# The first layer of an attention plus two-network kernel: seven block products of summed operands in place of eight

## The reference: what is computed

```python
# attention: q, k, v are (2, 8, 768, 64), proj is (64, 6)
mask = q_bucket[:, :, :, None] == k_bucket[:, :, None, :]     # buckets from signs of q @ proj, k @ proj
scores = where(mask, scale * q @ k.T, -1e9)
attn = exp(scores - max) / (sum + 1e-9)
x = (attn @ v) as 1536 tokens of 512
# first network: w1, w2 (512, 1024), w3 (1024, 1024), w_out (1024, 512)
x = ((x @ w1) * (x @ w2)) @ w3 @ w_out
# second network: w_gate, w_val (512, 1536), w_out (1536, 512)
out = (sigmoid(x @ w_gate) * (x @ w_val)) @ w_out
```

## Time and profile before

| | us |
|---|---|
| median of 3 runs (lowest, highest) | 790.92 (788.36, 793.75) |
| the profiled execution | 791.71 |
| its span, first to last instruction | 789.9 |
| busy in the span: PE, weight loads, DVE, ACT, POOL | 761.5, 699.9, 445.5, 426.1, 293.2 |
| matmuls | 4232 |
| mean granted clock of TensorE | 0.991 of full |

### The profile page before, as it was taken

One profiled execution on the slowest core, in us unless ns is written; L12 is line 12 of the kernel. 1 busy time (PEld: TensorE's weight loads), 2 busy tenths in 40 slices (PEclk: granted clock), 3 DMA queues, 4 the chain that ended last, 5 costly groups with the idle time before them and its releaser, 6 DMA issues.

```text
span 789.9 us, 12696 instructions
## 1 busy us (share of the span) xinstructions
PE 761.5 (96%) x4232; PEld 699.9 (89%) x4232; DVE 445.5 (56%) x995; ACT 426.1 (54%) x793; POOL 293.2 (37%) x203
## 2 busy tenths in 40 slices
PE   7889999999999988999999999999999999999998
PEld 4677878888797887999999999999999999988886
DVE  5879999999999997522222202534424415673100
ACT  5767888888888897423323323363453354624100
POOL 3777273645537243211112350024464464050000
PEclk9899999999999999999999999999999999999999
DMA  6592634435372600010000010001011010401101
GB/s 163 181 192 64 154 102 112 127 87 145 73 182 54 149 29 27 28 54 27 27 0 0 27 54 0 1 1 54 27 28 51 27 46 8 159 1 54 40 27 40
DMA packets 24653, 51.76 MB, mean 66 GB/s; under 512 B 3592, under 2 KB 9352, under 8 KB 24624
## 3 DMA queue, kind: packets, MB, share of 16 engines
q1 hardware_dynamic: 24400, 51.32, 24.1%
q10 hardware_dynamic: 224, 0.07, 0.0%
HBM read 29.43 MB, written 3.15 MB: 41 GB/s over the span
## 4 chain that ended last, share of the span: by engine, by line
PE 74%; DVE 10%; issue 5%; ACT 4%; DMA 3%; SPq 1%; POOL 1%; DVEq 0%; ACTq 0%; POOLq 0%
PE pair_bank L1183 12%; PE pair_bank L1184 12%; PE pair_bank L1185 12%; PE bank L1184 7%; PE bank L1183 7%; PE bank L1185 7%; PE bank L1108 5%; PE bank L1093 4%; PE pair_bank L1081 3%; DVE pt_lo L861 3%; DVE rowmax L828 3%; ACT pt_hi L550 2%; DVE prob L853 1%; DMA qk_raw<-in_qk 1%; DMA sq<-q_codes 1%
## 5 line engine op out<-in xcount | busy, mean ns | idle before, releaser
L861 DVE TENSOR_TENSOR pt_lo<-bank,pt_hi 128x384 fp32r<-128x384 f32 x192 | 97.6, 549 | 13.9 <-ACT pt_hi L550 13.6
L550 ACT ACTIVATE pt_hi<-bank 128x384 fp32r<-128x384 f32 x192 | 84.7, 488 | 34.7 <-PE bank L1093 33.4
L1093 PEld LDWEIGHTS bank<-ident,prob 128*128 128x128 f32 x576 | 67.4, 142 | 34.7 <-DVE pt_lo L861 14.5
L1093 PE MATMUL bank<-ident,prob 128*128 128x128 f32 x576 | 83.6, 280 | 14.8 <-DVE pt_lo L861 14.0
L568 ACT ACTIVATE prob<-pair_bank,ebias,escale 128x768 f32<-128x768 f32 x96 | 95.3, 992 | 4.2 <-DVE ebias L839 4.2
L1081 PE MATMUL pair_bank<-mk,sq 128*128 128x384 f32 x384 | 89.2, 354 | 5.5 <-DMA sq<-q_codes 3.0
L828 DVE TENSOR_REDUCE rowmax<-pair_bank 128x1 f32<-128x768 f32 x96 | 90.9, 947 | 4.3 <-PE pair_bank L1081 4.2
L1183 PE MATMUL pair_bank<-operand_hi,g_hi 128*128 128x384 f32 x240 | 80.3, 334 | 0.8 <-ACT u L550 0.8
L1185 PE MATMUL pair_bank<-operand_hi,g_lo 128*128 128x384 f32 x240 | 80.2, 334 | 0.0
L1081 PEld LDWEIGHTS pair_bank<-mk,sq 128*128 128x128 f32 x384 | 64.7, 190 | 15.2 <-issue 12.9
L444 POOL TENSOR_TENSOR w_lo<-w_raw,w_hi 128x512 fp32r<-128x512 f32 (+1 forms) x24 | 40.6, 1693 | 98.2 <-ACT w_hi L550 96.9
(11 more groups left out here) (163 smaller groups left out, 1963.7 us busy)
## 6 DMA issues: line engine op xcount, KB each, us to landing
sq<-hl SPq DMA_DIRECT2D x45, 192.0 KB
w_raw<-in_w SPq DMA_DIRECT2D x32, 256.0 KB, 2.8
mk<-hl SPq DMA_DIRECT2D x15, 384.0 KB
qk_raw<-in_qk SPq DMA_DIRECT2D x7, 768.0 KB, 5.3
v_raw<-in_v SPq DMA_DIRECT2D x16, 192.0 KB, 2.7
wo_raw<-in_wo SPq DMA_DIRECT2D x12, 256.0 KB, 3.9
out<-out_sb SPq DMA_DIRECT2D x12, 256.0 KB, 2.0
mk<-hl SPq DMA_DIRECT2D x15, 192.0 KB
```

Source lines behind the costliest of these rows:

```text
L550: return act.activation(dst, src, ACT.Copy)
L861: dve.tensor_tensor(pt_lo[(k // UQ) % 2][cut], t_bank[j][:, 0:384].rearrange("p (t n) -> p t n", t=3), pt_hi[(k // UQ) % 2][cut].bitcast(F ...
L1093: mm = pe.transpose(t_bank[j][:, 128 * t:128 * t + 128], prob[k % 3][:, 128 * (3 * j + t):128 * (3 * j + t) + 128], ident[:, :])
```

## The change

Layer 1 goes by the same seven products. Its eight groups are four pairs (`PAIRS1`), for `w1` and `w2`: eight units more, numbered 0 to 7, before layer 3's twelve. The helpers of layer 3 (`product`, `unit`, `kept`, `pair_weights`, `load_pair`) serve both. ACT's gate function is a plain copy in layer 1.

- The attention output `x_f` is now cut in blocks: B11 is pairs 4 and 5, B12 pairs 0 and 1 (T3 is made in its place), B22 pairs 2 and 3, B21 pairs 6 and 7. POOL makes T3 (two instructions of 128x768, one for each side) in the last but one pair, T2 and T1 in the last, DVE makes T4 after it.
- POOL also makes the first unit's weight sums (in the last but one pair) and their low part, its raw weights' low part and the high and low parts of B11 and the high part of T3 in the last pair. ACT makes that unit's high parts in steps 8 and 9 of the last but one pair, and three high parts of T2 and T1 in steps 9, 10 and 11 of the last. Gone are POOL's 128x1536 `x_hi` and `x_lo`, its split of the first 128x1024 weights, and ACT's 128x1024 `w_hi` at step 8 of the last pair.
- `h` stands whole in float32 (`h_f`). It is split only after its last piece, in six pieces: for the first chunk 128x2304 and 128x768, for the others 128x3072, high part by ACT (`h_high`), low part by DVE (`h_low`).
- In the last unit of layer 1 (7) ACT makes two high parts of `wp` between its `u1` and `u2` copies.
- The tiles of gate times value are three of 4 slices in place of one of 8 and one of 4, so their splits are 36 instructions of 128x512 on each engine, where 12 of 128x1024 and 12 of 128x512 were. ACT's and DVE's layer 3 loops are written out.

The core of the diff:

```diff
+X_HI_ORDER = ((T2, 0), (T2, 1), (T1, 0), (T1, 1), (B22, 0), (B21, 0), (B22, 1), (T4, 0), (B21, 1), (T4, 1))
+X_LOW_ORDER = ((T3, 0), (T3, 1), (T2, 0), (T1, 0), (T2, 1), (T1, 1), (B22, 0), (B22, 1), (B21, 0), (B21, 1),
+               (T4, 0), (T4, 1))
+PAIRS1, PAIRS3 = KF // 2, KF2 // 2
...
@@ POOL, pair(p, ...)
+                    else:
...
+                        x_sum(T2, T3, B11, ALU.add)
+                        pool.wait_ge(x_sums_done, 4)
+                        x_sum(T1, B22, T2, ALU.subtract)
                     attention_sum(p, 1)
                     v_split(p, 1)
+                if ahead:
+                    pool.wait_ge(x_done, PAIRS)
+                    for side in range(2):
+                        pool.tensor_tensor(x_raw(T3, side), x_raw(B22, side), x_raw(T3, side),
+                                           ALU.subtract).then_inc(x_sums_done, 1)
+                    pair_sums(0, 0)
...
-                    rounded(x_hi[:, 0, :, :], x_f[:, 0:KX, 0:HALF]).then_inc(x0_hi_done, 1)
-                    w_split(0, U1, w_raw[0][:, :])
-                    pool.wait_ge(x0_hi_done, 1)
-                    pool.tensor_tensor(x_lo[:, 0:KX, 0:HALF], x_f[:, 0:KX, 0:HALF],
-                                       x_hi[:, 0, :, :].bitcast(F32), ALU.subtract).then_inc(x0_split, 1)
+                    pair_raw_low(0, 0)
+                    for side in range(2):
+                        rounded(x_high(B11, side), x_raw(B11, side)).then_inc(x_hi_early, 1)
...
@@ ACT, pair(p, ...) and layer 1
-                    if last and k == 8:
-                        w_high(0, U1 + 2, w_raw[0][:, :], 1024, (fill_half, PAIRS))
+                    if ahead and k == 8:
+                        pair_raw_high(0, 0)
+                    if ahead and k == 9:
+                        pair_sums_high(0, 0)
+                    if last and k >= STEPS - 3:
+                        x_operand_high(*X_HI_ORDER[k - STEPS + 3])
...
+            unit(ACT.Copy, PAIRS1 - 1, 1, u_x, behind_first=((wp_high, 0), (wp_high, 1)),
+                 behind_last=((h_high, 0, 0, 6), (h_high, 0, 6, 8)))
...
@@ PE
-            layer1(0, 1)
-            with pe.Fori(1, KF // 2) as i:
-                for j in range(2):
-                    layer1(i, j)
+            unit(0, 0, x_high, x_low, x_operand, tuple((values, PAIRS - 1, 3, part) for part in range(3)))
+            unit(0, 1, x_high, x_low)
+            with pe.Fori(1, PAIRS1) as i:
+                for j in range(2):
+                    unit(i, j, x_high, x_low)
```

More of the change, by code:

```diff
@@ L47 @@
 L2_ORDER = (0, 2, 1, 3)
-L2_POS = (0, 2, 1, 3)
+H_AT = (140, 164, 152, 176)
 CH = 512
@@ new lines, in h_high @@
+            def h_high(pos, first_kt, last_kt):
+                c = L2_ORDER[pos]
+                rows = (v12_done, v22_done) if c < 2 else (v11_done, v21_done)
+                for done in rows:
+                    act.wait_ge(done, 2 * ((last_kt - 1) // 2) + c % 2 + 1)
+                act.wait_ge(*((y2_mm, L1_LAST), (y4_mm, L1_LAST), (x2_mm, KX), (x2_mm, 2 * KX))[pos])
+                copy(h_hi[pos % 2][:, first_kt:last_kt, :], h_f[c][:, first_kt:last_kt, :]).then_inc(h_hi_done, 1)
+            unit(ACT.Copy, 0, 1, u_x)
@@ L808, in _ @@
             for t in (4, 5):
-                gv_high_a(t)
-                gv_high_b(t)
+                for part in range(3):
+                    gv_high(t, part)
             for t in range(TT):
@@ L818, in _ @@
                 if t + 6 < TT:
-                    gv_high_a(t + 6)
-                    gv_high_b(t + 6)
+                    for part in range(3):
+                        gv_high(t + 6, part)
         @block.vector
@@ L953, in _, with add @@
-            layer1(0, 0)
-            layer1(0, 1)
-            with dve.Fori(1, KF // 2) as i:
+            dve.wait_ge(x_tmp_done, 4 * PAIRS)
+            attention_out(slice(D, 2 * D), 1, pv_bank[D:2 * D, 0:HALF])
+            x_sum4(1)
+            for q, side in X_LOW_ORDER[4:10]:
+                x_operand_low(q, side)
+            def add(mm, kept_sem, n, acc, src, done):
+                dve.wait_ge(mm, n + 1)
+                dve.wait_ge(kept_sem, n + 1)
+                dve.tensor_tensor(acc, src, acc, ALU.add).then_inc(done, 1)
@@ L1196, in layer1_chunk, with product @@
-            def layer1_chunk(i, j, c):
-                tok = slice(HALF * (c % 2), HALF * (c % 2) + HALF)
-                two_products(j, (mlp[c][0][:, 0:HALF], mlp[c][1][:, 0:HALF]),
-                             lambda kt: (x_hi[:, c, kt, :], x_lo[:, KX * (c // 2) + kt, tok]))
-            def layer1(i, j):
-                pe.wait_ge(w_ready[j], U1 + i + 1)
-                for c in range(L1C):
-                    pe.wait_ge(product_done, L1C * (2 * i + j - 1) + c + 1)
-                    layer1_chunk(i, j, c)
+            def product(j, weight, high, low, dst, start, done):
+                lo = g_raw_lo[j][:, weight, :] if weight < S1 else g_sum_lo[j][:, weight - S1, :]
+                for kt in range(2):
+                    cols = slice(128 * kt, 128 * kt + 128)
+                    mm = three(dst, g_hi[j][:, weight, cols], lo[:, cols], high[:, kt, :], low[:, kt, :],
+                               start=(start and kt == 0), stop=(kt == 1), partial=True)
+                mm.then_inc(done, 1)
```

832 lines of the change are left out of this document (430 added, 402 removed).

## The result

The changed kernel took 778.7 us (median of 4 runs, 775.4 to 781.17); the kernel before took 789.64 us (787.87 to 793.75). The ratio is 0.9857, with an interval of 0.9822 to 0.9891. The forecast was 779 us, between 773 and 788. Ten runs of the changed kernel over the whole study have a median of 780.1 us.

The account below looks back on a forecast made before the run. The number of matmuls was taken to set layers 1 and 3, with PE and DVE both nearly full in attention. Terms -16.7 + 1.0 + 2.5 + 1.3 = -11.9 us led from a 790.92 median to 779 us, range 773 to 788.

Parts of the forecast that it names:

- Step 1: Layer 1: 96 fewer matmuls at 0.1736 us each, all on the path, -16.7 us.
- Step 2: Attention's last two pairs: `x_lo` and `w_hi` go, new POOL and ACT work costs; +1.0 us, between -5.5 and +32.
- the ratio 0.077: Attention: DVE time lost per microsecond of POOL work; 27.7 us of new POOL work costs 2.1 us.
- ACT's inserts: Attention's last two pairs: ACT's new high parts of weights and operands, 4.4 us, half counted: 2.2 us.
- Step 3: Into layer 1: weight sums 0.8 late, DVE low parts meeting POOL 1.7; +2.5 us, between 0.8 and 8.2.
- just in time: First unit of layer 1: T4's low part ready at 14.1 us from PE's start, wanted at 14.6.
- Step 4: Out of layer 1: `u2` 0.7 us late, first split of `h` 0.6; +1.3 us, between 0.7 and 6.0.
- Step 5: Layer 3 and output: matmuls and unit order as before; 0, with 0.5 us to either side.
- The fourth: Attention's last two pairs: POOL's new instructions hold DVE for most of their length; slower, in full 806 us; chance 0.05.
- The third rival: Seams take most of the gain: way in 5.5, way out 3, attention +3; 783 to 799 us; chance 0.19.

Follow-up runs that it names:

- halves: Changed kernel with POOL's sums of x, parts of B11 and high part of T3 in instructions of 384 columns, not 768: 780.55 us, ratio 0.9869.
- The two edits: Changed kernel, T4's low part ahead of DVE's c22 additions, POOL waiting for eight x parts before pair (1,1)'s low weight parts: 775.81 us, ratio 0.9819.
- the changed kernel's second: Profile from the changed kernel run again unchanged, 6 runs: 781.56 us, ratio 0.9877.
- T4 earlier: Changed kernel with DVE's low part of T4's x moved ahead of its additions for c22: 777.01 us, ratio 0.9827.
- the matmuls given back: Changed kernel with twelve more matmuls into a free bank in each of seven of layer 1's eight units: 793.86 us, ratio 1.0038.

## Why the prediction was right

The median of 779 was met to 0.3 us, and by the step of the sum it was met in this way:

```
us                              forecast   measured
1 matmuls removed                -16.7      -16.6
2 attention's last two pairs      +1.0       -1.2
3 into layer 1                    +2.5       +5.6
4 out of layer 1                  +1.3       +1.4
5 layer 3 and output               0         -1.0
sum                              -11.9      -11.8
```

The sum is the profile's 17.0 less the 5.2 of the start. Some of the agreement is luck: terms 2 and 5 were too high by 3.2 us together, and term 3 too low by 3.1. The start and the lower clock are in no term, and the median of ten runs, 780.1, is a microsecond above the forecast. The kernel before had 789.64 us in these runs and not the 790.92 that the forecast started from: the medians moved by 10.9 us, where 11.9 was forecast.

**Step 1 held.** I had 0.1736 us a matmul and the traces say 0.1733; 684 of them are 118.6 us of layer 1 after, and 84 given back cost 14.55. The middle units are 14.56 us apart, as forecast.

**Step 2** missed its sign, +1.0 for -1.2. POOL's new work cost the path 2.3 us (steps 13 to 95), and the forecast from the ratio 0.077 was 2.1. That agreement is partly luck: the ratio prices DVE's time, and the sixteen scalings of the last two pairs took 3.7 us more (16.0 for 12.3, with the 3.64 us one counted at 0.62), not all of it on the path. `x_lo` and `w_hi` gave back 3.5, forecast 3.25, but not in those shares. With `x_lo` in pieces and `w_hi` still in place, the kernel before takes 7.34 us from step 95 to layer 1, and the changed kernel 7.59: `x_lo` was worth all of it, where I had counted half its price, 2.3, and no gain from `w_hi` (0.95) is seen. ACT's inserts were priced at 2.2, half of their length, because `w_hi` had been in the chain of waits. From step 80 to step 84, where ACT rounds the first weight sums, it took 11.78 us before and 11.81 after. Of the 2.3 us, 1.1 come between steps 79 and 80, behind the 1.97 us scaling, and 1.3 between 84 and 95, of which halves took back 0.9: at most 0.4 is left for ACT's other inserts. An engine that is once in the chain isn't full; I should have read its idle time there.

**Step 3** is the term that was mis-sized: 125.61 - 118.6 - 1.4 = 5.6 us, within its bounds of 0.8 to 8.2. It named the main cause rightly (low parts on DVE meeting POOL's weights). Its other part, 0.8 us for the second unit's weight sums, did not come: PE has no wait for them. The reckoning "just in time" for T4 was off, since it had no meeting in it. Two meetings lay on the path (3.30 for 1.83, 3.99 for about 1.9), each pause cost about 0.3 us more than its row says (314.96 stands 2.98 behind the start before it, in place of 0.17, for a wait of 2.65, and the next start is 0.28 behind), a third pause of 0.3 lay before 322.68, and the first wait had 1.4 us of DVE's own queue in it, which no term held. The two edits take 2.8 us of it away.

**Step 4** was right: waits of 0.4 us for `u2` (0.7 forecast) and 0.6 for the split of `h` (0.6 forecast), and 1.4 us from start to start.

**Step 5** took the wait of 0.8 us in the earlier trace rows, which lay at 665 us in layer 3's last unit but one, for fixed. Ahead of it ACT waited 2.20 us for POOL's `g_sum`, and now 1.15, so the copy `u` is in time. POOL's last two sums there took 1.71 and 1.60 us before and 1.19 and 1.06 after. I had not asked what stood ahead of that wait.

**The signs.** Three that the prediction named went against it. PE's first product was to be at 311 to 313 us and came at 304.63, or at 309.9 with the 5.24 us of the start put back, since attention gained where it was to lose. Layer 1 was to take 122.5 us and took 125.61. And a drop of the granted clock in layer 1 was to be a sign of being wrong: the first profile has none, but the second has one, with 1.5 us.

**The rivals.** The fourth, DVE held for POOL's length, did not come: 2.3 us of 27.7, and the scalings in the last two pairs average 1.00 us, not over 1.3. Its mechanism is real, and the Trainium skill (SBUF — State Buffer, "Who interferes with whom") describes it: the later of a DVE instruction that takes the shared ports and a GpSimd instruction waits for the whole of the other. By that rule cutting POOL's instructions in two should cut the loss, and the trace of the halves agrees, with 1.3 us. It does not say how often two meet; that came from the ratio. The third rival, seams that take most of the gain, put the way in at 5.5 us and was right there, and with the lower clock behind a pause in four of the nine profiles; it was wrong on attention and the way out.

What the times hold beyond the sum: outside the span (the time less first to last instruction) the changed kernel takes 2.4 to 2.6 us in every run, the kernel before 1.8. These 0.7 us are not explained.

## What to carry to other kernels

Price removed matmuls by start-to-start time and look for the payment where the operands of the new scheme first come in: a chain that is "just in time" on paper is late by the meetings of DVE and GpSimd on it, 1.3 and 2.1 us for the two here. Put a two-input low part on DVE before GpSimd's next long instruction, or let GpSimd wait, and cut GpSimd's long instructions where DVE's short ones are on the path (1.3 us here by the trace, not shown by the times). When an early transfer decides the start of a run, compare stretches from the first steady step on; the span alone would have put 5.2 us of the start down to the change.

## What was not expected of the hardware

The granted clock after a pause. After PE pauses of 3.33 us (twice) and 2.49 us it fell to the lower level in every profile; after the pause of 2.63 to 2.65 us in three profiles (the changed kernel's second, T4 earlier, halves; ten matmuls or so, 0.32 us apart), and not in two (the changed kernel's first, the matmuls given back); after 1.69 to 1.73 us in none of thirteen, after 1.41 us in none of three, and after 0.90 us not in the one. With the pauses before step 12 it fell in all eight profiles where they were 1.88 to 3.26 us long, and in neither of the two with 1.16 and 1.38. The same pause at the same place did both, and 1.88 us did it in one place where 2.64 did not in another, so the length alone does not decide. An edit that shortens such a pause may gain these 1.5 us beside the pause.

The start. The first steady step of attention came anywhere from 52.56 to 58.55 us in twelve profiles, three with the old first layer (56.59 to 58.29) and nine with the new. Most of that lies between steps 11 and 13, which took 5.0 us where the transfer into `sq` was in time and 6.3 to 9.8 where it was late, with the lower clock behind it in eight of those ten.
